# An expert stage with its weights as the stationary operand, in 31 slots of 64 tokens

## What is computed

```python
logits = np.einsum('bsd,de->bse', x, w_gate)
local_gate = 1.0 / (1.0 + np.exp(-np.einsum('bsd,de->bse', x, w_local).squeeze(-1)))
for b in range(B):
    prev_e = -1
    for s in range(S):
        fresh_e = int(np.argmax(logits[b, s]))
        e = fresh_e if s == 0 or local_gate[b, s] < 0.5 else prev_e
        prev_e = e
        p = softmax(logits[b, s])
        h = np.maximum(x[b, s] @ w1[e], 0.0)        # 512 -> 1024
        out[b, s] = p[e] * (h @ w2[e])              # 1024 -> 512
```

## Time and profile before

| | |
|---|---|
| median of the runs | 564.95 us (563.42 to 566.49) |
| profiled execution | 567.09 us, of which its span is 565.1 |
| TensorE matmul / weight load busy | 493.5 (87%) / 303.4 (54%) us |
| VectorE, ScalarE, GpSimd busy | 291.7, 291.0, 335.8 us |
| attention | to about 268 us |
| routing | about 268 to 312 us |
| expert stage | about 312 us to the end |
| TensorE share of the chain that ended last | 59% |
| matmuls / weight loads | 4,348 / 4,348 |

### The profile page before, as it was taken

The page is one execution under the profiler, slowest core; times in us unless marked ns, Lnnn a source line. Parts: engine busy times, 40 slices in busy tenths (PEclk is TensorE's granted clock), DMA queues, the critical chain, the costliest instruction groups (busy, mean ns, idle before and its releaser), DMA issues.

```text
span 565.1 us, 11139 instructions
## 1 busy us (share of the span) xinstructions
PE 493.5 (87%) x4348; PEld 303.4 (54%) x4348; DVE 291.7 (52%) x415; ACT 291.0 (51%) x267; POOL 335.8 (59%) x175
## 2 busy tenths in 40 slices
PE   4679999999999999986821769999999999999984
PEld 2335777676767676765620345555555555555531
DVE  4466666666666666521856241554544545454440
ACT  4258787878787878765250500094865957000000
POOL 1336687878787878796301985078968769400010
PEclk9979999999999999988555678999999999999997
DMA  7935545555336331000910137346383461200000
GB/s 236 188 116 147 145 133 159 144 145 154 80 70 190 70 79 42 18 1 1 351 61 11 45 113 186 108 192 231 124 313 120 194 257 61 83 13 20 6 0 0
DMA packets 55842, 65.12 MB, mean 115 GB/s; under 512 B 31395, under 2 KB 39983, under 8 KB 55794
## 3 DMA queue, kind: packets, MB, share of 16 engines
q1 hardware_dynamic: 52754, 56.29, 32.7%
q0 software_dynamic: 3040, 8.13, 4.7%
HBM read 47.99 MB, written 8.13 MB: 99 GB/s over the span
## 4 chain that ended last, share of the span: by engine, by line
PE 59%; POOL 13%; ACT 9%; DVE 8%; issue 5%; DMA 3%; SPq 2%; ACTq 0%; POOLq 0%; DVEq 0%
PE pA L1025 18%; PE pO L1025 18%; POOL room L399 8%; ACT room L561 5%; POOL W L291 4%; PE pB L1043 3%; ACT room L567 3%; PE pA L458 2%; PE pA L459 2%; DMA room<-room 2%; PE pP L1015 2%; PE pB L475 2%; PE pB L476 2%; DVE room L640 1%; PE pA L835 1%
## 5 line engine op out<-in xcount | busy, mean ns | idle before, releaser
L399 POOL TENSOR_TENSOR room<-room 128x1536 f16<-128x1536 f32 x48 | 148.8, 3101 | 44.6 <-ACT room L567 44.4
L291 POOL TENSOR_TENSOR W<-room,W 128x1024 f16<-128x1024 f32 x64 | 135.0, 2133 | 42.1 <-ACT W L283 41.9
L277 ACT ACTIVATE room<-W 128x1024 f32<-128x1024 f32 x64 | 64.7, 1049 | 100.3 <-DMA W<-in_moe_w 69.3
L640 DVE TENSOR_REDUCE room<-pA 128x2 f32<-128x1536 f32 x46 | 80.9, 1758 | 55.1 <-PE pA L459 55.0
L1025 PE MATMUL pA<-W,room 128*128 x456 | 104.4, 385 | 3.2 <-DVE room L1093 2.1
L1025 PE MATMUL pO<-W,room 128*128 x456 | 104.2, 386 | 2.7 <-DVE room L1105 2.7
L561 ACT ACTIVATE room<-pB 128x1536 f32<-128x1536 f32 x48 | 69.4, 1446 | 39.7 <-PE pB L476 37.4
L1025 PEld LDWEIGHTS pA<-W,room 128*128 128x128 f16 x456 | 45.0, 99 | 55.6 <-issue 7.9
L1025 PEld LDWEIGHTS pO<-W,room 128*128 128x128 f16 x456 | 45.4, 99 | 54.6 <-issue 6.5
L567 ACT ACTIVATE room<-room 128x1536 f16<-128x1536 f32 x48 | 71.3, 1485 | 1.5
L513 PE MATMUL pO<-W,room 128*128 128x64 f16 x576 | 63.8, 194 | 3.3 <-POOL room L399 3.3
(11 more groups left out here) (185 smaller groups left out, 649.0 us busy)
## 6 DMA issues: line engine op xcount, KB each, us to landing
W<-in_moe_w SPq DMA_DIRECT2D x32, 1024.0 KB, 7.5
room<-room SPq DMA_DIRECT2D x96, 96.0 KB, 3.2
room<-in_q SPq DMA_DIRECT2D x16, 192.0 KB, 3.2
room<-in_k SPq DMA_DIRECT2D x16, 192.0 KB, 3.3
W<-in_v SPq DMA_DIRECT2D x4, 768.0 KB, 8.0
x_rows<-XN SPq DMA_DIRECT2D x12, 256.0 KB, 3.2
room<-room SPq DMA_DIRECT2D x32, 18.0 KB
room<-room SPq DMA_DIRECT2D x32, 1.5 KB
```

Of the source, the lines that this page charges most:

```text
L291: pool.tensor_tensor(parts(r)[:, 1, cols], FULL[:, place(r), cols], parts(r)[:, 0, cols], ALU.subtract).then_inc(s_ready, 1)
L399: pool.tensor_tensor(PTL[:, n % NP, :, :], E32[:, n % 2, :, :], PTH[:, n % NP, :, :], ALU.subtract).then_inc(s_lo, 1)
L640: dve.reduce_max(RM[:, g % 2, 2 * p:2 * p + 2], scores_in(n)[:, :].rearrange("p (i s) -> p i s", i=2), AX.X).then_inc(s_rmax, 1)
```

## The change

- Weights are stationary. In `up` the stationary operand is a 128x128 block of w1 (high or low part) and the moving one 64 columns of transposed tokens; the result is already transposed (pH, 1024 hidden x 64 tokens in 8 blocks), so `ht` and its fp32 transposes go. `down` does the same with w2 and gives the output transposed (pYT), so a pair of slots is turned back by `turn_y`, four transposes.
- 31 slots of 64 tokens (1,536 / 64 + 8 - 1) in place of 19 tiles of 128. Gathers, `xt`, `turn_y`, gates and scatters work on 16 pairs of slots.
- `up` and `down` have 96 matmuls each per slot, every one with a weight load of its own. The offset is taken into one view of W by `weights(t)`, out of which the slices are cut.
- VectorE's `hc` has three passes over 128x512 per slot: relu in place in PSUM, high part, low part; `ytc` copies pYT to SBUF; hidden buffers and X are doubled.
- The gates are split into three float16 parts (GP) and brought to the order of the pairs by 12 float16 matmuls with the one-hot rows that the map already uses (ROWH); ROWOH and the fp32 matmuls go.
- The loads of expert e + 3 wait for `s_yt`, the end of `down` of expert e's last slot. Tables have 31 columns (TC, TF, TI) or 16 (BY, FROM, TO).

The core of the diff:

```diff
-    NT = T // P + E - 1
+    HT = 64
+    NK = T // HT
+    SLOTS = NK + E - 1
+    PR = (SLOTS + 1) // 2
...
-                sp.wait_ge(s_ht, ends[e] + 1)
+                sp.wait_ge(s_yt, ends[e])
...
-            def product(o, hi, lo, k, at, n):
-                cols = slice(k * P, (k + 1) * P)
-                wh, wl = W[:, bass.ds(at, 512)], W[:, bass.ds(at + CHUNK, 512)]
-                for m, (l, r) in enumerate(((hi, wl), (lo, wh), (hi, wh))):
-                    last = pe.matmul(o, l[:, cols], r, start=k == m == 0, stop=k == n - 1 and m == 2)
-                return last
+            def weights(t):
+                return W[:, bass.ds(tab(0, t, 0, PARTS * (RING - 1)), PARTS)]
 
             def up(t):
-                off = tab(0, t, 0, PARTS * (RING - 1))
+                w, q, cols = weights(t), t // 2, slice(t % 2 * HT, t % 2 * HT + HT)
                 pe.wait_ge(s_ready, tab(1, t, 8, 8 * E))
-                pe.wait_ge(s_xc, t + 1)
-                wait(pe, s_hs, t)
-                for n in range(F // 512):
+                pe.wait_ge(s_xc, q + 1)
+                wait(pe, s_hc, t - 1)
+                for f in range(FC):
                     for d in range(DC):
-                        at = off + (d // (DC // 2) * 4 * CHUNK + d % (DC // 2) * F + n * 512)
-                        last = product(pH[:, n * 512:(n + 1) * 512], XH, XL, d, at, DC)
+                        at = d // (DC // 2) * 4 * CHUNK + d % (DC // 2) * F + f * P
+                        wh, wl = w[:, at:at + P], w[:, at + CHUNK:at + CHUNK + P]
+                        for m, (l, x) in enumerate(((wl, XH), (wh, XL), (wh, XH))):
+                            last = pe.matmul(pH[t % 2][:, f * HT:(f + 1) * HT], l, x[:, q % 2, d, cols],
+                                             start=d == m == 0, stop=d == DC - 1 and m == 2)
                 last.then_inc(s_h, 1)
...
             def down(t):
-                off = tab(0, t, 0, PARTS * (RING - 1))
+                w, q, side = weights(t), t // 2, t % 2
                 pe.wait_ge(s_hc, t + 1)
-                wait(pe, s_yc, t)
-                for f in range(FC):
-                    at = off + ((f // (FC // 2) * 4 + 2) * CHUNK + f % (FC // 2) * DM)
-                    last = product(pY[:, 0:DM], HH, HL, f, at, FC)
-                last.then_inc(s_y, 1)
+                wait(pe, s_ytc, q)
+                for c in range(DC):
+                    o = pYT[:, c * P + side * HT:c * P + (side + 1) * HT]
+                    for f in range(FC):
+                        at = (f // (FC // 2) * 4 + 2) * CHUNK + f % (FC // 2) * DM + c * P
+                        wh, wl = w[:, at:at + P], w[:, at + CHUNK:at + CHUNK + P]
+                        for m, (l, x) in enumerate(((wl, HH), (wh, HL), (wh, HH))):
+                            last = pe.matmul(o, l, x[:, side, f, :], start=f == m == 0, stop=f == FC - 1 and m == 2)
+                last.then_inc(s_yt, 1)
+
+            def turn_y(q):
+                pe.wait_ge(s_ytc, q + 1)
+                wait(pe, s_yc, q)
+                for d in range(DC):
+                    last = pe.transpose(pY[:, d * P:(d + 1) * P], YT[:, d, :], idf[:, :])
+                last.then_inc(s_y, 1)
 
             xt(0)
             up(0)
+            for t in range(SLOTS):
+                if t + 1 < SLOTS:
+                    up(t + 1)
+                if t == 0:
+                    pe.wait_ge(s_by, 2)
+                    for c in range(NC):
+                        last = pe.matmul(pT[0][:, 0:3 * PR], ROWH[:, c, :], BG[:, c, :, :].rearrange("p a t -> p (a t)"),
+                                         start=c == 0, stop=c == NC - 1)
+                    last.then_inc(s_map, 1)
+                if t % 2 == 0:
+                    if t > 0:
+                        turn_y(t // 2 - 1)
+                    if t // 2 + 1 < PR:
+                        xt(t // 2 + 1)
                 down(t)
+            turn_y(PR - 1)
...
+            def hc(t):
                 dve.wait_ge(s_h, t + 1)
-                wait(dve, s_ht, t)
-                dve.tensor_scalar(HS, pH[:, 0:F], 0.0, HSC / (XS * WS), ALU.max, ALU.mult).then_inc(s_hs, 1)
+                wait(dve, s_yt, t - 1)
+                h, s = pH[t % 2].rearrange("p (f n) -> p f n", f=FC), HSC / (XS * WS)
+                dve.tensor_scalar(h, h, 0.0, None, ALU.max).then_inc(s_relu, 1)
+                dve.wait_ge(s_relu, t + 1)
+                dve.tensor_scalar(HH[:, t % 2, :, :], h, s, None, ALU.mult).then_inc(s_hhi, 1)
                 dve.wait_ge(s_hhi, t + 1)
+                dve.scalar_tensor_tensor(HL[:, t % 2, :, :], h, s, HH[:, t % 2, :, :],
+                                         ALU.mult, ALU.subtract).then_inc(s_hc, 1)
+            def ytc(q):
+                dve.wait_ge(s_yt, min(2 * q + 2, SLOTS))
+                wait(dve, s_y, q)
+                dve.tensor_copy(YT[:, :, :], pYT[:, :].rearrange("p (d n) -> p d n", d=DC)).then_inc(s_ytc, 1)
```

More of the change, by code:

```diff
@@ L699, in lsh_attention_moe_kernel @@
         low_at = Layout(full_at.at)
[L700 to L707, removed]
+        XIN = low_at.take(PR, DM)
+        HH = low_at.take(2, FC, HT, dt=f16)
+        HL = low_at.take(2, FC, HT, dt=f16)
+        XH = low_at.take(2, DC, P, dt=f16)
+        XL = low_at.take(2, DC, P, dt=f16)
+        YT = low_at.take(DC, P)
+        XTC = XIN[:, PR - 2:PR, :].rearrange("p t n -> p (t n)").bitcast(f16).rearrange("p (c a n) -> p c a n", c=2, a=2)
         def rt(shape, dt):
@@ L723, in lsh_attention_moe_kernel @@
         RT = rt([P, 2, B, J], fp32)
-        ROWS = XIN[0:B, NT - 7:NT - 2, :].rearrange("b t n -> b (t n)")[:, 0:3 * S].rearrange("b (a n) -> b a n", a=3)
+        ROWS = XIN[0:B, PR - 7:PR - 2, :].rearrange("b t n -> b (t n)")[:, 0:3 * S].rearrange("b (a n) -> b a n", a=3)
         EB = rt([P, B, J], fp32)
         GATE = rt([P, NC], fp32)
+        GP = low_at.take(NC, 3, dt=f16)
+        SG = rt([P, PR], fp32)
         TS = small(E, NC)
@@ L730, in lsh_attention_moe_kernel @@
         restart = rt([P, E, NC], fp32)
-        CMP = small(E, NC)
+        CMP = small(E, NK)
         TL = rt([P, E], fp32)
@@ L760, in lsh_attention_moe_kernel @@
         eid8 = rt([P, E], fp32)
-        k128 = rt([P, NC], fp32)
+        first = rt([P, NK], fp32)
         s_rt = sem("s_rt")
@@ L927, in _ @@
             dve.wait_ge(s_map, 1)
[L928 to L933, removed]
@@ L997, in _ @@
                 low_weights(pool, r, 1)
-            for t in range(3, NT):
-                gather(t)
+            for q in range(3, PR):
+                gather(q)
+            done = 0
             for e in range(RING, E):
                 low_expert(e)
-                for t in range(0 if e == RING else e, NT if e == E - 1 else e + 1):
-                    scatter(t)
-            pool.wait_ge(s_out, 16 * NT)
+                ready = PR if e == E - 1 else (e + 1) // 2
+                for q in range(done, ready):
+                    scatter(q)
+                done = ready
+            pool.wait_ge(s_out, 16 * PR)
         @block.tensor
@@ L1056, in _ @@
             up(0)
-            xt(1)
-            ht(0)
-            up(1)
-            pe.wait_ge(s_by, 2)
-            for c in range(NC):
-                last = pe.matmul(pT[0][:, 0:NT], ROWOH[:, c, :], BG[:, c, :], start=c == 0, stop=c == NC - 1)
-            last.then_inc(s_map, 1)
-            xt(2)
-            down(0)
-            ht(1)
-            for t in range(1, NT - 2):
-                up(t + 1)
-                xt(t + 2)
-                down(t)
-                ht(t + 1)
-            up(NT - 1)
-            down(NT - 2)
-            ht(NT - 1)
-            down(NT - 1)
+            for t in range(SLOTS):
[12 more added lines that the diff above has]
+                        xt(t // 2 + 1)
+                down(t)
+            turn_y(PR - 1)
         @block.scalar
```

178 lines of the change are left out of this document (89 added, 89 removed).

## The result

The changed kernel took 934.72 us (median of two runs, 932.85 to 936.59) against 564.95: a ratio of 1.654, with a 95% interval of 1.646 to 1.663. The profiled execution took 932.85 us for a span of 931.1. The forecast was 893, so the direction and the cause were foreseen and 38 us of the size were not.

A forecast was written before the change was run, and what follows sets the result against it. TensorE's matmuls bound the kernel before; its queue, issuing address instructions, would bind after. 314.6 us before the stage, 571 for 31 slots of 18.4, less 1.3, plus 8.8 of tail gave 893 us; range 850 to 990.

The forecast's parts named there:

- The count of addresses: In `up` and `down`: one address instruction for each weight place in a register, 128 a slot, 3,968 in all.
- The step: TensorE's queue in the expert stage: address instructions start 0.125 us apart, 16.0 us a slot; bounds 0.046 and 0.127.
- Value loads and waits: TensorE's queue, each slot: three table value loads of 0.65 us plus 0.5 us of semaphore waits, no longer hidden.
- Stalls of the queue: TensorE's queue: stalls between blocks of instructions, twice as many to bring in, could take the time up to 930 us.
- The clock: TensorE in the expert stage: granted clock may fall to 0.5 without effect, 0.165 us a product against 0.25 of issue.
- The gates: Front of the expert stage: 11 us of fp32 one-hot and passes leave the chain, already in the sum, no extra term.
- VectorE: Its passes take 3.5 us a slot, hidden under 18.4, and under 6.2 if the array were the bound.
- Loads bound: Rival, expert stage: weight loads from register addresses follow 0.11 us apart, hiding the queue; 992 us, chance 0.09.
- three addresses: Rival, expert stage: an address for every load, 192 a slot, 26.5 us a slot, 1,144 us; chance 0.05.
- One address a product: Rival, expert stage: 10.4 us a slot, 645 us; chance 0.05, shared with a step near 46 ns.
- Addresses free: Rival, expert stage: no instruction between the load and matmul pairs, 520 us, alone faster than before; chance 0.07.
- Weights: Expert weight loads: 25.9 us from issue to last subtraction, six slots ahead of first use, so no wait.

## Why the prediction was right, and where it was off

*The count of addresses* was right to the last one: 3,968, no fewer for `weights(t)` asking once and none for the second use of `wh`.

*The step* was mis-sized, the largest error: 0.125 was read off 16 and 13 instructions in the earlier trace rows, 0.132 is the mean over thousands. None of those 27 steps is over 0.135 us (the 0.127 came of the rounding of 1.9 us), so the rows held not one of the longer steps that are every eighth in the changed kernel. Nothing in them could have shown it; why they had none is open. 3,968 x 0.132 = 524 us stand where 496 did: +28.

*Value loads and waits* were right: 2.45 us a slot forecast, 19.3 less 128 x 0.132 leaves 2.4. A value load is worth 0.66 us by its removal. A slot was 19.3 us instead of 18.4, all of it from the step.

*Stalls of the queue* were in the range ("stalls of the queue between blocks") and not in the sum. They cost about 12 us, once, from 331 to 346 us, and not between blocks but beside the gathers, whose issue the prediction counted as hidden with "16 gathers and scatters for 19". The 12 us are the time from the end of `up(1)` to that of `down(0)`, 21.5 us (331.6 to 353.2), less the 9.5 of the kernel with three gathers there (329.7 to 339.2). 893 + 28 + 12, less 1.4 for a stage that starts at 313.2 instead of 314.6 us, is 932; the span is 931.1. The tail behind the last `down` is 8.7 us for 8.8.

*The clock* fell to 0.55 and nothing followed from it, as forecast; the kernel with more work for the array shows it.

*The gates* cost nothing on the path, as forecast, since `down(0)` is issued behind 9 us of `up(1)`. Their size was not foreseen. VectorE's timeline in the changed kernel, with GpSimd's last subtraction of the low parts:
```profile
324.14 1.03 DVE L1133 TENSOR_SCALAR room<-room 128x12 f32<-128x12 f32 x1
325.21 0.23 DVE L1134 RECIPROCAL room<-room 128x12 f32<-128x12 f32 x1
325.47 1.87 DVE L1135 TENSOR_TENSOR room<-room 128x96 f32<-128x96 f32 x1
...
325.10 2.13 POOL L296 TENSOR_TENSOR W<-room,W 128x1024 f16<-128x1024 f32 x1
```
The product over 96 elements took 0.26 us in the kernel before, where GpSimd issued gathers and subtracted nothing; here it takes 1.87 and ends at 327.34, 0.11 after GpSimd's instruction (327.23). The 1.03 us of the one before end at 325.17, 0.02 after the subtraction before that one. The Trainium skill, SBUF — State Buffer, in its terms and its section on the two sides, says that VectorE and GpSimd take a shared pair of ports by an exclusive lock for a whole instruction, and that the loser blocks. The trace agrees: the small instructions end with the large one. With the array as the bound this is on the path: four such instructions take 6.9 us instead of 0.8 in the kernel of fixed addresses, some 6 of the 8 us of its gates.

*VectorE* was hidden at 19.3 us a slot, as forecast. For the case of an array-bound stage the same claim failed: 3.5 us of work fit under 6.2, but their order does not, and 12 times `up` came some 0.7 us late. A share of busy time was used where the order on the queue decides.

*The rivals.* Loads bound, 992 us, is 61 us from the result (the forecast was 38 off), so the time alone does not exclude it well; one, two and three addresses (675, 931, 1,175 us of span) do. One address a product came at 675.4 for 645, three at 1,174.8 for 1,144; both miss by 30 us, in the same direction as the forecast and for the most part by the step (11.23 us a slot for 10.45, 27.5 for 26.5). Addresses free came at 550.8 for 520, with the three parts named above; of these the stops of the queue for late instructions were in no part of the forecast. The step from which it would decide, 42 ns, was never near: 132.

*Weights* never came late, in the changed kernel or with fixed addresses, where expert 3's loads go out at 345.5 us, its low parts are ready at 371.5 (26.0 us for the 25.9 of the forecast) and its first `up` starts at 394.6.

## What to carry to other kernels

An operand whose place is held in a register costs TensorE's queue one instruction for every distinct place, 0.132 us here; so count the addresses of a stage against the array's time between them before operands are made smaller, and read the step off some hundred of them where the queue sets the pace, not off a dozen. Here 512 moving columns hid two addresses (0.25 under 0.65 us), 64 columns did not (0.25 over 0.09). If the places can be constants, do that first. Before a part on the path is made cheaper, see whether it can be moved off: the cheap gates alone gained nothing, moved behind `down(0)` they gained 2%. And look at more than one engine's queue before a gap of "issue" is explained.

## What was not expected of the hardware

- Address instructions step at 0.124 us and about every eighth one takes some 0.06 to 0.08 more, whatever stands between them (472 of 3,968, 485 of 3,968, 244 of 1,984, 730 of 5,952), but none of 27 read in the kernel before.
- GpSimd's gathers can go with a stop of TensorE's and VectorE's queues: 12 steps in 10.8 us beside 13 of them, none beside three, and the stop moves with them; but beside the same 13, one every 1.25 us, there is none with one or three addresses a product or with fixed ones.
- A block of TensorE's instructions came late eight times beside weight loads, and the queue ran dry for 0.6 to 3.0 us each time.
- Small VectorE instructions (12 to 96 elements a partition) took 1.0 to 2.1 us instead of 0.17 to 0.26 while GpSimd subtracted in SBUF.
- 87% busy matmuls and 70% busy weight loads on the profile's page of a kernel whose array had work for about half of the time in the steady stage (10.6 of 19.3 us), at a clock of 0.55.
